# Attention with a low-rank mix and an MLP on one core: the slots of a batch's mixing inside the next batch's attention

## The reference

```python
# attention: B=4 batches, H=8 heads, S=576 positions, D=64
q_rot, k_rot = rotate(q), rotate(k)                    # rotary embedding
attn = softmax(q_rot @ k_rot.T / sqrt(D))
x = (attn @ v), heads side by side: (B, 576, 512)
# mixing over the positions, rank 32, then the MLP
h = (x.T @ U) @ V ;  u = x + h.T
out = u + relu(u @ w_ch1) @ w_ch2                      # w_ch1: 512 x 2048
```

## Time and profile before

| | us |
|---|---|
| three runs | 798.22, 800.57, 799.39 |
| median | 799.39 |
| profiled execution | 799.79, of which the span from first to last instruction 797.7 |
| busy over the span: TensorE, VectorE, ScalarE, GpSimd | 725.8, 373.0, 373.4, 260.1 |
| mean granted TensorE clock | 0.987 of full speed |

### The profile page before, as it was taken

The page is one execution under the profiler, slowest core; times in us unless marked ns, Lnnn a source line. Parts: engine busy times, 40 slices in busy tenths (PEclk is TensorE's granted clock), DMA queues, the critical chain, the costliest instruction groups (busy, mean ns, idle before and its releaser), DMA issues.

```text
span 797.7 us, 11651 instructions
## 1 busy us (share of the span) xinstructions
PE 725.8 (91%) x4336; PEld 655.4 (82%) x4336; DVE 373.0 (47%) x619; ACT 373.4 (47%) x807; POOL 260.1 (33%) x182
## 2 busy tenths in 40 slices
PE   0799998989898989987499999999999999999998
PEld 0689887778787878775499999999999999999997
DVE  2689897788778897786411121121212112122112
ACT  1689998789878989774433211111210111111100
POOL 6667758556866658300455200000000000000000
PEclk9999999999999999999799999999999999999999
DMA  7856665577457753523763030011003003001001
GB/s 239 237 147 188 174 189 139 152 225 197 127 164 227 205 164 90 130 70 119 219 243 128 1 119 1 0 61 59 1 1 118 1 1 119 0 1 40 1 1 39
DMA packets 45942, 86.47 MB, mean 108 GB/s; under 512 B 7552, under 2 KB 20032, under 8 KB 43840
## 3 DMA queue, kind: packets, MB, share of 16 engines
q1 hardware_dynamic: 45456, 84.50, 35.9%
q10 hardware_dynamic: 432, 1.25, 0.4%
HBM read 43.25 MB, written 14.16 MB: 72 GB/s over the span
## 4 chain that ended last, share of the span: by engine, by line
PE 50%; DVE 1%; ACT 0%; issue 0%; DVEq 0%
PE ps L842 25%; PE ps L855 25%; DVE utl L802 1%; DVE res L809 0%; ACT wh L777 0%; DVE wl L813 0%; DVEq L808 0%
## 5 line engine op out<-in xcount | busy, mean ns | idle before, releaser
L819 DVE SCALAR_TENSOR_TENSOR htl<-ps,hth 128x384 fp32r<-128x384 f32 x96 | 53.5, 558 | 325.8 <-ACT hth L794 325.8
L794 ACT ACTIVATE hth<-ps 128x384 fp32r<-128x384 f32 x96 | 47.2, 492 | 328.1 <-PE ps L842 328.1
L496 DVE TENSOR_REDUCE negmax<-ps 128x1 f32<-128x576 f32 (+1 forms) x160 | 120.2, 751 | 55.1 <-PE ps L602 53.7
L602 PE MATMUL ps<-stack 128*128 128x288 f32 (+1 forms) x640 | 125.3, 319 | 22.3 <-DMA stack<-raw 22.3
L842 PE MATMUL ps<-uth,wh 128*128 128x384 f32 x384 | 130.1, 339 | 10.1 <-DVE utl L802 10.1
L412 ACT ACTIVATE prob<-ps,negmax 128x576 f32<-128x576 f32 (+1 forms) x160 | 118.4, 740 | 41.8 <-DVE negmax L496 40.9
L842 PE MATMUL ps<-uth,wl 128*128 128x384 f32 x384 | 130.0, 338 | 0.0
L842 PE MATMUL ps<-utl,wh 128*128 128x384 f32 x384 | 129.5, 337 | 0.0
L502 DVE TENSOR_TENSOR ptl<-ps,pth 128x512 fp32r<-128x512 f32 (+1 forms) x192 | 121.4, 646 | 3.6 <-ACT pth L421 1.9
L855 PE MATMUL ps<-wl,hth 128*128 128x512 f32 x288 | 114.0, 396 | 0.0
L620 PE MATMUL ps<-ident,prob 128*128 128x128 f32 (+1 forms) x672 | 97.7, 270 | 17.7 <-ACT prob L412 16.1
(11 more groups left out here) (65 smaller groups left out, 860.4 us busy)
## 6 DMA issues: line engine op xcount, KB each, us to landing
stack<-raw SPq DMA_DIRECT2D x192, 144.0 KB, 2.6
raw<-in_qk SPq DMA_DIRECT2D x16, 1152.0 KB, 5.5
tables<-in_w SPq DMA_DIRECT2D x11, 512.0 KB, 4.5
raw<-scratch_ut SPq DMA_DIRECT2D x6, 768.0 KB, 6.7
res<-scratch_u SPq DMA_DIRECT2D x18, 256.0 KB, 3.5
out<-res SPq DMA_DIRECT2D x18, 256.0 KB, 2.1
vraw<-in_v SPq DMA_DIRECT2D x16, 256.0 KB, 5.3
scratch_u<-xn SPq DMA_DIRECT2D x16, 256.0 KB, 3.2
```

Source lines behind the costliest of these rows:

```text
L496: nc.vector.tensor_reduce(negmax[0:w, n % NT:n % NT + 1], scores_of(n, w), AX.XY, ALU.max, negate=True).then_inc(maxed, 1)
L602: mm = nc.tensor.matmul(ps[0:w, at_:at_ + CH], stack[:, r % 2, i, 0, P * t:P * t + w], stack[:, r % 2, i, part, CH * c:CH * c + CH], start ...
L794: nc.scalar.activation(hth[:, i % 2], up_bank(i), ACT.Relu).then_inc(relu_hi, 1)
L819: nc.vector.scalar_tensor_tensor(htl[:, i % 2], up_bank(i), 0.0, hth[:, i % 2], ALU.max, ALU.subtract).then_inc(relu_lo, 1)
```

## The change

Only the table of slots changes. The first two natural items keep their slots. The other naturals stand one to three slots earlier, the low-rank product in slot 16 instead of 21, the residual and transposed items in slots 18 to 30 instead of 23 to 38, and two slots (23 and 26) hold one residual and one transposed item each. The order of the sixteen items among themselves is the same as before. MIX_END, the number of slots after the attention, follows the table and is 32 instead of 40.

```diff
-MIX_AT = {6: [("natural", 0)], 8: [("natural", 1)], 11: [("natural", 2)], 13: [("natural", 3)],
-          16: [("natural", 4)], 21: [("low_rank", 0)], 23: [("residual", 0)],
-          26: [("residual", 1)], 27: [("transposed", 0)], 28: [("residual", 2)],
-          30: [("transposed", 1)], 31: [("residual", 3)], 33: [("residual", 4)], 34: [("transposed", 2)],
-          36: [("transposed", 3)], 38: [("transposed", 4)]}
+MIX_AT = {6: [("natural", 0)], 8: [("natural", 1)], 10: [("natural", 2)], 11: [("natural", 3)],
+          13: [("natural", 4)], 16: [("low_rank", 0)], 18: [("residual", 0)], 20: [("residual", 1)],
+          21: [("transposed", 0)], 23: [("residual", 2), ("transposed", 1)], 25: [("residual", 3)],
+          26: [("residual", 4), ("transposed", 2)], 28: [("transposed", 3)], 30: [("transposed", 4)]}
```

## The result

| | before | after |
|---|---|---|
| median of ten runs, us | 799.58 | 803.36 |
| lowest to highest | 798.22 to 800.87 | 800.60 to 804.58 |
| profiled execution, us | 799.79 | 800.93 |
| its mean granted clock | 0.987 | 0.994 |

A forecast was written before the change was run, and what follows sets the result against it. Attention was taken as bound by saturated engines with none free for mixing; all terms were 0 except the nine items, 3 x 0.2 = 0.6 us, giving 800.0 beside the median of 799.39, range 796.8 to 803.8.

The forecast's parts named there:

- rival B: Ring of banks: five additional one-slot releases cost in full as VectorE falls behind, 1.1 us a batch, 803.3; chance 0.25.
- slots 60 to 70 near 25.8: Sign of being right: the dense block's eleven slots take near 25.8 us in the profile after.
- 86.5 to 88 us between the exponentials: Sign of being right: exponentials of slots 40 and 80 still 86.5 to 88 us apart.
- the mean clock moved: Sign of being wrong: a mean granted clock that moved from 0.987.
- What bounds it: Attention: no free engine for mixing to fall into, so it lengthens attention anywhere; 16.46 us a batch.
- Tail: Behind slot 160: same instructions in the same order, the eight slots fewer are empty; cost 0, gain 0.
- Naturals at nothing, their stalls under the idle stretch: Slots 50, 51, 53: new stalls fit under TensorE's 2.43 us idle; 0 per batch, up to 1.0 if not hidden.
- GpSimd's margin of 0.9 us: GpSimd's low parts done at 134.47, low-rank product needs them at 135.3: ahead by 0.9 us, cost 0.
- Low rank and residual 0: Slots 56 and 58 instead of 61 and 63: again t=1 and t=3 with a pv slot between; cost 0.
- The nine items at 0.2 per batch, upper end 1.0: Residual 1 to transposed 4 in slots 60 to 70: 0.2 us per batch, ends -0.4 and +1.0.
- slots 62, 64, 67, 69 as slot 69, 2.21 each: Dense block: four slots with a pv and no item, priced like slot 69 before, 8.84 us together.
- Rival A: Slot-52 stall: shorter TensorE idleness keeps the clock at 2.4 GHz, 1 to 1.8 us per fall saved, 797.0; chance 0.2.

The follow-up runs named there:

- e6: Kernel before with natural 1 in slot 10, low rank in 18 and the residual and transposed items respaced for the ring: 789.54 us against 800.23, ratio 0.9869.
- e8: Kernel before with only naturals 2, 3 and 4 moved to slots 10, 11 and 13: 796.87 us against 800.23, ratio 0.9969.
- e1: Kernel before with naturals 2 to 4, low rank and residual 0 in the change's new slots, later items unmoved: 797.68 us against 798.84, ratio 0.998.
- e2: Kernel before with only residual 1 to transposed 4 packed into slots 25 to 35, two slots holding two items: 803.45 us against 798.84, ratio 1.0055.
- e5: Kernel before with low rank, residual and transposed items respaced for four one-slot releases instead of six: 796.07 us against 800.23, ratio 0.9953.
- e3: Changed kernel with its two double slots undone, residual 1 to transposed 4 one to a slot in 20 to 33: 798.78 us against 798.84 before, ratio 0.9992.
- e7: Changed kernel with VectorE's pv addition and splits ahead of its row maximum in five slots per batch: 807.86 us against 800.23 before, ratio 1.0106.
- e4: Kernel before with only natural 1 moved from slot 8 to slot 10: 790.17 us against 798.84, ratio 0.9885.

## Why the prediction was right or wrong

The time lay inside the range, 3.4 us over the forecast by medians and some 2 by the ratio. The forecast of no change did not hold: the kernel is slower by just over 0.3%, and the median lies above the forecast's own range of 798.3 to 802.4, in the slower part (over 801.8) to which I had given 0.27. The width of the range, made for rival B, held the time, not the forecast's mechanism. Of the signs, slots 60 to 70 near 25.8 failed (26.47), and so did 86.5 to 88 us between the exponentials (88.22), and the mean clock moved. Point by point:

- *What bounds it.* Right in the main: the attention has no free engine. But the 16.46 us per batch were not all work: e6 runs the same items with 2.96 us less, by placement alone. Behind the block, slots 71 to 79 ran nearly bare: 16.25 us for nine, bare 15.86.
- *Tail.* Right. The loads for phase B went out 13.6 us earlier by the trace (347.93 instead of 361.50), and phase B began at nearly the same distance behind the attention, 27.6 us from slot 159's exponential to ScalarE's first instruction there, 27.9 before.
- *Naturals at nothing, their stalls under the idle stretch.* Right: 0.17 and 0.81 us were there, TensorE's wait fell to 1.55 (1.9 forecast), and e8 measured -0.15 per batch.
- *GpSimd's margin of 0.9 us.* Right: 0.9, and no wait of the low-rank product for it.
- *Low rank and residual 0.* Right in sum: e1, which moves them and the naturals, is 0.01 off before.
- *The nine items at 0.2 per batch, upper end 1.0.* Here it failed, by size: 1.28. The step that was mis-sized is "slots 62, 64, 67, 69 as slot 69, 2.21 each". I had listed the turned tiles of slots 64 and 67 among the eleven one-slot releases and then priced them with a template, slot 69 before, that holds no such wait. They measured 2.68 and 2.70, 0.96 together over the template; slots 62 and 69 were 0.24 over it. Slot 68 was 0.56 under its template, which had held an old wait of 0.35 for ScalarE's copy of a transposed item. With smaller differences that makes 26.47 for 25.82, 0.65 over. The copy of transposed 4, left out of the sum of slots and allowed for in the 0.2, measured 0.39 over bare slots, and slots 40 to 59 took 0.13 more. In TensorE's timeline before, the template's old wait:

```profile
181.87 0.46 PE L656 MATMUL ps<-ident,xn 64*128 64x64 f32 x4 [0.35 <-ACT uts L446]
```

- *Rival B* named this place and its price (1.1 per batch, turned tiles of 64 and 67 waiting), and its time of 803.3 is close to the median. That closeness is partly luck: without the gain by the clock the median would have been over 804, and its own sign, slots 60 to 70 over 26.6, was just missed with 26.47. Its reason, VectorE falling behind, was wrong: VectorE idles for the scores; it is its order, not its load. The rule of the Trainium skill that it rested on (Perfetto Trace Analysis, Optimization Strategy: consistent bubbles can mean too little SBUF or PSUM for the next tile) points the right way here: the repeated waits of 0.81 and 0.20 are for banks of a full ring. Whether a larger ring would end them was not tried.
- *Rival A* came true at the same time, which I had not allowed: I priced the two as alternatives. At 0.994 the profiled run had no fall in the attention, other runs went down to 0.989, before 0.985 to 0.989. I had priced a saved fall at 1 to 1.8 us; at the stall it is worth 0.7. (In slots 80 to 119 before takes 87.71 us with a fall, e1 87.02 without.) I had also overlooked the third fall of the profile before, at 41.6 us, outside the part that the change touches. Schedule +3.8 and clock about -1.1 make the 2.7 of the ratio. The second is only the difference; e1, with an unchanged schedule, gained 1.2 by the medians and 1.6 by the ratio.

## What to carry to other kernels

In a software pipeline with a small ring, write out who frees each bank and how many slots lie between. A release within one slot costs TensorE up to 0.8 us here behind a turned tile and up to 0.97 behind a pv. In slot 64 the freeing engine first waited for that very slot's input. Putting two items in a slot shifted such releases onto the main stream's own tiles. Their number alone is no price: e1 and e8 have eight, before six, and cost nothing more per batch. When an item is moved, price every tenant behind it, not the moved item alone. And look at the in-order queue of the engine that seems idle: the largest gain here, 6.5 us of schedule plus the clock, was one small GpSimd instruction that waited ahead of work that was ready.

## What the hardware showed that was not expected

The granted clock is a term of the schedule, and not the same in each run. In the attention's slots each fall lasts 3.4 us at 1.2 GHz. It costs 0.7 us in slots 52 to 56 and some 1.6 in the bare slots 7 to 10 of the first batch (39.3 to 39.5 us from slot 0 to slot 20 in the five profiled executions that have it, 37.5 to 38.1 in the five that do not).

The ten profiled executions show what TensorE did before. Where it had stood idle for 2.4 us in slot 53 of a batch (before, e2, e5) the clock fell beside it in 7 of 9 batches. With 1.54 to 1.60 us there (after, e1, e3, e7, e8) it fell in none of 15, and in e4 and e6, without that stall, in none of 6. In the first batch every kernel has the same instructions and an idle stretch of 2.06 to 2.18 us in slot 8, and 5 of 10 executions have a fall there: whether that one comes does not hang on the table of slots. One more fall, in e7, follows three short waits of 1.02, 0.20 and 0.25 us in one double slot.

Over all runs the picture is similar but less clean. With TensorE idle for 2.43 us in slot 53 the mean clock of before's runs was 0.985 to 0.989; with 1.55 us (e1, e8) 0.988 to 0.994; with that stall gone (e4) 0.991 to 0.993, and four runs within 0.8 us. Two kernels stand across this: e5 kept the 2.43 us and had 0.986 to 0.991, e7 had 1.56 us and 0.987 to 0.989. So an idle stretch that ScalarE would have hidden anyway can still be worth shortening, and a single profiled execution (800.93, clock 0.994) can lie 2.4 us from the median of the same kernel.
